# A fused attention, experts and feed-forward kernel: other orders in step 1 and of block sums, first weights loaded last, queries in one piece per head

## The reference

```
# attention: 2 sequences, 8 heads, 768 positions, 64 features
k_sum = k.reshape(B, H, 24, 32, D).max(axis=3)      # one summary key per block of 32
v_sum = v.reshape(B, H, 24, 32, D).mean(axis=3)
scores_l = scale * q @ k.T, where |i - j| < 16, else -1e9
scores_s = scale * q @ k_sum.T + log(32)
a = softmax(concat(scores_l, scores_s)); x = a @ concat(v, v_sum)
# four experts, 1536 tokens, 512 features, 1024 hidden
p = probs / (probs.sum(-1) + 1e-9)
x = sum_e p[:, e] * (relu(x @ w1[e]) @ w2[e])
# feed-forward, 2048 hidden
h = x @ w_in; out = (h * sigmoid(1.702 h)) @ w_out
```

## Time and profile before

| | us |
|---|---|
| three executions | 844.20, 845.85, 846.78 (median 845.85) |
| the profiled execution | 845.02 |
| its span | 843.2 |
| TensorE busy in it | 818.9 (97%) |
| VectorE / POOL / ACT busy | 542.0 / 555.5 / 399.1 |

### The profile page before, as it was taken

How to read it: one execution, slowest core, us unless ns; L and a number is a source line. 1 busy time by engine, 2 the same in 40 slices (tenths; PEclk the granted TensorE clock), 3 DMA queues, 4 the chain that set the end, 5 groups by cost and what they waited for, 6 DMA issues and landing times.

```text
span 843.2 us, 13851 instructions
## 1 busy us (share of the span) xinstructions
PE 818.9 (97%) x5014; PEld 805.1 (95%) x5014; DVE 542.0 (64%) x1194; ACT 399.1 (47%) x859; POOL 555.5 (66%) x414
## 2 busy tenths in 40 slices
PE   5896999999999999999999999999999999999998
PEld 4786999999999999999999999999999999999998
DVE  6896666656665566566566666666676665665665
ACT  3863544544444454434334344444455555454541
POOL 3685566656566699756656578877578887466450
PEclk9978999999999999999999999999999999999999
DMA  9981216142112112212213112112112112322102
GB/s 265 277 218 57 92 54 216 51 149 73 51 63 108 51 51 93 77 51 98 72 51 108 62 51 101 51 50 101 51 51 101 50 55 96 126 68 84 51 1 76
DMA packets 26420, 74.72 MB, mean 89 GB/s; under 512 B 14704, under 2 KB 15856, under 8 KB 20208
## 3 DMA queue, kind: packets, MB, share of 16 engines
q1 hardware_dynamic: 26352, 73.84, 26.9%
HBM read 70.66 MB, written 3.17 MB: 88 GB/s over the span
## 4 chain that ended last, share of the span: by engine, by line
PE 89%; POOL 3%; SPq 3%; issue 1%; DMA 1%; DVE 1%; ACT 1%; DVEq 0%; ACTq 0%; POOLq 0%
PE bank L1146 29%; PE bank L1148 29%; PE bank L1147 29%; DMA v_cols<-v_t 1%; PE bank L1101 1%; SPq L404 1%; PE bank L1138 1%; PE bank L1112 1%; SPq L411 1%; POOL wd_lo L543 0%; POOL wd_lo L559 0%; POOL xb_other_lo L567 0%; POOL w_sum L520 0%; SPq L422 0%; SPq L417 0%
## 5 line engine op out<-in xcount | busy, mean ns | idle before, releaser
L948 DVE TENSOR_TENSOR xa<-bank,xa 128x384 f32<-128x384 f32 x352 | 195.8, 557 | 220.0 <-PE bank L1148 215.6
L1146 PE MATMUL bank<-h_hi,wd_hi 128*128 128x384 f32 x768 | 257.8, 336 | 0.1
L1148 PE MATMUL bank<-h_lo,wd_hi 128*128 128x384 f32 x768 | 257.4, 335 | 0.0
L1147 PE MATMUL bank<-h_hi,wd_lo 128*128 128x384 f32 x768 | 257.3, 335 | 0.0
L543 POOL TENSOR_TENSOR wd_lo<-stage,wd_hi 128x1024 fp32r<-128x1024 f32 x47 | 112.5, 2393 | 169.1 <-ACT wd_hi L714 169.1
L755 ACT ACTIVATE h_hi<-bank 128x384 fp32r<-128x384 f32 x192 | 94.3, 491 | 226.0 <-DVE bank L981 178.7
L1146 PEld LDWEIGHTS bank<-h_hi,wd_hi 128*128 128x128 f32 x768 | 144.7, 188 | 1.2 <-issue 1.2
L1147 PEld LDWEIGHTS bank<-h_hi,wd_lo 128*128 128x128 f32 x768 | 144.7, 188 | 0.0
L1148 PEld LDWEIGHTS bank<-h_lo,wd_hi 128*128 128x128 f32 x768 | 144.7, 188 | 0.0
L531 POOL TENSOR_TENSOR wu_lo<-stage,wu_hi 128x1024 fp32r<-128x1024 f32 x47 | 112.6, 2396 | 0.0
L1146 PE MATMUL bank<-xb_other_hi,wu_hi 128*128 128x384 f32 x336 | 112.3, 334 | 0.3 <-ACT snap L739 0.3
(11 more groups left out here) (79 smaller groups left out, 1283.2 us busy)
## 6 DMA issues: line engine op xcount, KB each, us to landing
stage<-weights SPq DMA_DIRECT2D x48, 1024.0 KB, 4.9
k_win<-k_w SPq DMA_DIRECT2D x8, 720.0 KB, 8.9
v_win<-v_w SPq DMA_DIRECT2D x8, 576.0 KB, 9.1
q_bd<-q_t SPq DMA_DIRECT2D x16, 192.0 KB, 8.8
p_bc<-p_rows SPq DMA_DIRECT2D x8, 384.0 KB, 4.8
v_cols<-v_t SPq DMA_DIRECT2D x6, 384.0 KB, 6.0
out<-xa SPq DMA_DIRECT2D x4, 384.0 KB, 7.5
out<-xa SPq DMA_DIRECT2D x8, 192.0 KB, 1.9
```

The source lines that it names most:

```text
L948: nc.vector.tensor_tensor(at, y_bank(g, t), at, ALU.add).then_inc(y_taken, 1)
L1146: nc.tensor.matmul(dst, w_h, a_h, start=first, stop=False, skip_group_check=True)
L1147: nc.tensor.matmul(dst, w_l, a_h, start=False, stop=False, skip_group_check=True)
L1148: return nc.tensor.matmul(dst, w_h, a_l, start=False, stop=last, skip_group_check=True)
```

## The change

**Queries in one piece.** `q_bd` is laid out as [partition, column, tile] in place of [partition, tile, column], and the host stores `q_t` likewise. A half is then 3072 bytes in one piece for each of 64 partitions, where it was twelve pieces of 256 bytes. The 128 columns of a tile, which the score matmul loads, now lie 12 words, 48 bytes, apart. The zeroing is of the same size.

**Weights.** `load_weights(0)` goes behind unit 3's value columns and windows.

**Value sums.** For units 1 to 3 `value_sums`, `turn_value_sums` and `value_means` come one slot later (`values_due`), the spread in the same slot as before.

**First blocks and weights.** `high_raw(0)` goes from slot 10 to 12, `high_down(0, .)` from 13 to 14; POOL's halves of `wu_lo` from slots 11 and 12 to 13 and 14, those of `wd_lo` from slots 14 and 15 to behind `low_sums(1)`.

**Step 1.** ACT takes `keep(1, 1)` before the exponentials of group 12 and `high_raw(2)` behind the hidden tile; VectorE does `low_moved(4)` before `add_c11` and `value_sums(4)` behind the first `take_y`.

```
-            q_bd[i] = sb(stack, f"q_bd{i}", [P, TILES, P])
+            q_bd[i] = sb(stack, f"q_bd{i}", [P, P, TILES])
...
+        def values_due(slot, lag):
+            return [u for u in range(KT) if slot - lag == GROUPS * u + L_SUM + (u > 0)]
...
-                    sp.dma_start(q_bd[at_set(u)][rows, :, DH * half:DH * (half + 1)],
-                                 q_t[u, rows, :].rearrange("p (t n) -> p t n", n=QT)).then_inc(q_in[at_set(u)], 16)
+                    sp.dma_start(q_bd[at_set(u)][rows, QT * half:QT * (half + 1), :],
+                                 q_t[u, rows, :].rearrange("p (n t) -> p n t", t=TILES)
+                                 ).then_inc(q_in[at_set(u)], 16)
...
-            load_weights(0)
             load_value_columns(3)
             load_value_windows(3)
+            load_weights(0)
...
-                for u in unit_starting(slot, L_MEAN + 1):
-                    if u == 0:
-                        spread_value_means(u, kwin_done, 2)
-                for u in unit_starting(slot, L_MEAN + 2):
+                for u in values_due(slot, 2):
                     if u:
                         spread_value_means(u, norm_done, slot - L_NORM + 1)
-                if slot in (11, 12):
-                    low_first(slot - 11)
-                if slot in (14, 15):
-                    low_first(slot - 12)
+                    else:
+                        spread_value_means(u, kwin_done, 2)
+                if slot in (13, 14):
+                    low_first(slot - 13)
...
+                if g == 0:
+                    low_first(2)
+                    low_first(3)
                 if g + 1 < STEPS:
                     low_down(g + 1)
...
-                for u in unit_starting(slot, L_MEAN):
+                for u in values_due(slot, 1):
                     value_means(u)
-                if slot == 10:
+                if slot == 12:
                     high_raw(0)
-                if slot == 12:
                     high_moved(0, 0)
                 if slot == 13:
                     high_moved(0, B12)
+                if slot == 14:
                     high_down(0, 0)
                     high_down(0, 1)
...
                     high_down(1, 1)
+                    keep(1, 1)
                     exponent(B_GROUPS)
+                    high_hidden(1, "C11")
+                    high_moved(0, 5)
+                    high_raw(2)
...
             sum_first(4)
+            low_moved(4)
...
                     take_y(0, 0)
-                    low_moved(4)
+                    value_sums(KT)
+                    take_y(0, 1)
                     low_hidden(1, "C11")
-                    take_y(0, 1)
                     invert_sums(B_GROUPS)
                     take_y(0, 2)
                     low_moved(5)
                     take_y(0, 3)
-                    value_sums(KT)
...
-                    last = nc.tensor.matmul(s_bank(k)[:, t * KEYS:(t + 1) * KEYS], q_bd[at_set(u)][:, t0 + t, :],
+                    last = nc.tensor.matmul(s_bank(k)[:, t * KEYS:(t + 1) * KEYS], q_bd[at_set(u)][:, :, t0 + t],
```

More of the change, by code:

```diff
@@ L486, in _ @@
             for s in range(SETS):
-                nc.gpsimd.memset(q_bd[s][0:DH, :, DH:P], 0.0).then_inc(q_zeroed, 1)
+                nc.gpsimd.memset(q_bd[s][0:DH, QT:P, :], 0.0).then_inc(q_zeroed, 1)
             def spread_key_maxima(u):
@@ L795, in _ @@
                     high_down(1, 1)
+                    keep(1, 1)
                     exponent(B_GROUPS)
[L797 to L803, removed]
-                        exponent(k)
[L805 to L809, removed]
+                    high_hidden(1, "C11")
+                    high_moved(0, 5)
+                    high_raw(2)
+                else:
+                    if more:
+                        high_raw(g + 1)
+                    if ffn:
+                        sigmoid(g, "C11")
+                    high_hidden(g, "C11")
+                    for k in step_group(g):
+                        exponent(k)
+                    for k in step_group(g - 1):
+                        take_x(k)
+                    keep(g, 1)
                 if more:
@@ L995, in _ @@
             for s in range(SETS):
-                nc.vector.memset(q_bd[s][DH:P, :, 0:DH], 0.0).then_inc(q_zeroed_low, 1)
+                nc.vector.memset(q_bd[s][DH:P, 0:QT, :], 0.0).then_inc(q_zeroed_low, 1)
             for slot in range(SLOTS):
@@ L1008, in _ @@
                     key_maxima(u)
-                for u in unit_starting(slot, L_SUM):
+                for u in values_due(slot, 0):
                     value_sums(u)
@@ L1319 @@
         "consts": constants(),
-        "q_t": features_first(q),
+        "q_t": np.ascontiguousarray(features_first(q).reshape(UNITS, P, TILES, QT).swapaxes(2, 3)).reshape(UNITS, P, SEQ),
         "k_w": np.pad(windows(k_rows), ((0, 0), (0, 0), (0, 0), (0, NBLK))),
```

## The result

| | before | after |
|---|---|---|
| four executions each, us | 844.20 to 846.78, median 845.61 | 857.15 to 858.49, median 857.75 |
| ratio after / before | | 1.0145, interval 1.0126 to 1.0163 |
| the profiled execution, its span | 845.02, 843.2 | 857.26, 855.5 |
| TensorE busy | 818.9 | 838.8 |
| DMA packets | 26420 | 15156 |

A forecast was written before the change was run, and what follows sets the result against it. TensorE bounds everything behind 100 us, so gains lie before, the largest in its 5.26 us hole at P7. Step 1 -6.7, attention -1.4, stride 0: -8.1 us, giving 837.8 us from the median 845.85, range 835.2 to 844.0.

The forecast's parts named there:

- R3: Score matmuls: a strided load takes four times the packed one, 220 ns; +5.9 us, 851.8 us, slower; chance 9%.
- (a): Step 1: with keep(1,1) ahead of the exponentials and block 4's low part earlier, TensorE's hole at P7 goes; -5.4 us.
- (b): Step 1: 18 matmuls after the hole run at 0.17 instead of 0.33 us if the clock stays up; -2.7 us.
- (c): Step 1: value_sums(4) behind the first take_y removes TensorE's wait for it; -1.5 us.
- (d): Step 1: new TensorE waits for VectorE's take_y and POOL's normalization; +2.9 us together, between 1.4 and 4.5.
- (e): Step 1: POOL's wd_lo halves moved behind low_sums(1) cost 0 with 2 us of cover, up to 2 if landing is slow.
- (h): Attention: load_weights(0) behind unit 3's values lets value columns land earlier and the sum no longer delay mask 9; -1.8 us.
- (g): Attention: value sums of units 1 to 3 one slot later; +0.7 us, between 0 and +1.9.
- (f): Attention: queries in one piece let the first value columns land earlier; -0.7 us, between 0 and -2.8.
- (i): End of attention: low_first(1) of wu_lo behind POOL's last normalization ends at 47.7 us, covered by 1 us.
- (j): First tiles, begun 1.8 us earlier, may run that long at half clock rate; +0.4 us, between 0 and +0.9.
- R1: The clock falls all the same, a late landing of (e) counted here; gain only -4.9 us, 841.0 us; chance 17%.

The follow-up runs named there:

- run 6: The kernel before with only the change's step 1 orders of ACT and VectorE; 838.30 us, ratio 0.9925.
- run 7: The kernel before with all of the change but the queries' layout and the step 1 orders; 845.46 us, ratio 1.0003.
- Run 9: The kernel before with the step 1 orders and load_weights(0) behind unit 3's values, high_raw(0) staying in slot 10; 838.42 us.
- run 8: The changed kernel with query columns 8 bytes apart and the value sums of units 1 to 3 back in their old slots; 838.14 us.
- run 11: Run 6's kernel plus POOL's normalization of group 12 ahead of low_raw(2); 835.63 us, ratio 0.9878.
- run 1: The changed kernel with the old, packed layout of the queries, all new orders kept; 838.25 us, ratio 0.9924.
- run 12: Run 1's kernel plus POOL's normalization of group 12 ahead of low_raw(2); 836.61 us, ratio 0.9887.
- run 5: The changed orders with query columns 12, 24, 4 and 48 bytes apart in the four query buffers; 848.29 us in a single execution.
- run 3: The changed kernel with tiles in pairs, query columns 8 bytes apart, pieces of 512 bytes; 838.57 us.

## Why the prediction was wrong

**The step that failed** is the cost of the strided load, in one sentence: "I take 0, because the nearest rows leave half of the pace free." The half was free: packed, 32 lines at 1.8 ns are 58 ns (an estimate), near the 55 that the prediction drew from the 64-column loads. But the stride multiplies that time by four and more, not by up to two. The bound above, 220 ns, was a fair account of words coming one at a time (231 ns at 16 bytes, 219 at 24) and too low for 48 bytes (263). So the truth lay outside both ends, with 152 ns over the pace instead of 109: 14.6 us behind 50 us instead of 10.5, and 5.4 in attention instead of 3.5 (the last by one trace of each). The prediction's own sign of being wrong came: the loads pace at 263 ns, over its 130. Rival R3 named the mechanism and got 9%; it crossed to the slower side from 174 ns on, and of the steps tried only 4 and 8 bytes stay below that. With no row for or against, the four-fold bound, the only value that followed from a mechanism, deserved more than 9%.

**Step 1** was right: -6.7 foreseen, 6.7 us in run 6. (a) holds: no wait for `snap` at P7. (b) holds: clock 1.00 from 60 to 80 us (0.75 from 55 to 60, as the first tile begins). (c) holds: no wait for `v_sum`. (d) had the right engines and the wrong shares: VectorE 0.7 us in two waits (2.2 foreseen in four), POOL's `prob` 1.4 (0.7 foreseen), together 2.1 against 2.9. The sum came out though its shares did not: from the scores of group 12 to those of group 13 run 6 takes 20.9 us where before took 27.4, 6.5 less, and (a), (b) and (c) are worth 9.6, so 3.1 us were lost anew; what the waits do not show lies in short gaps beside them. In the changed kernel the waits are 0.2 and 1.4, since VectorE has 1.2 us more while TensorE loads group 12. (e) cost nothing: TensorE waits from 55 us to the end for VectorE's `xa`, POOL's `prob` and one `snap`, for no weights, and POOL's sums of step 2 do not wait for `stage`.

**Attention**, -1.4 foreseen, gave nothing: run 7 has 845.46 against 844.98. (h), -1.8, is not in run 7's time, though VectorE's wait for value columns at 34 us is gone there: its first tile starts at 49.66 us, between the 50.52 and 48.36 of the old orders. Before, that wait does stand in the chain of work that ended last, so the prediction had a path right; what it left out is that another must be about as long. Which one was not followed up. Run 9 adds little here, since its edit makes ACT wait 2.47 us for the weights. (g), +0.7, is not measurable (run 8). (f), -0.7: the packets came out (15156), and VectorE begins the first sum at 8.76 us in place of 9.47 in the changed kernel. That is no gain there, since TensorE leads, and within scatter: with the old layout it began at 9.24 in run 9 and 9.08 in run 11. Here one trace is worth little: the first tile starts at 50.52 us in the profiled execution of before and at 48.36 in that of run 6, whose instructions up to there are the same. (i) looked at the second half of `wu_lo` only. The first now stands ahead of the last normalization and holds it up: 3.8 us between the last two in place of 2.5 (the rows under the result, and the same in runs 1 and 7), with TensorE waiting 2.35 us behind. The move also frees earlier slots, and no run has the halves of `wu_lo` alone in their old slots, so what it costs in sum is open; it may be a part of what attention did not gain. (j) is within the scatter of the first tile's start and stays open.

The sum without the stride, -8.1, measured -6.3 (run 1), and R1 did not come.

From the first tile to the scores of group 13 the changed kernel and run 1 take 32.07 us alike, although the strided block of group 12 adds 1.2 us. VectorE's waits give back 0.5 (0.7 to 0.2), and the short gaps beside them about as much again: all that TensorE's starts between the two groups' scores lie over their 0.174 us pace is 3.2 us in run 1 and 2.2 in the changed kernel, the waits counted. The last 0.2 us is within the scatter.

## What to carry over

Lay out a stationary operand so that at least two of its 4-byte columns share 16 bytes, and cost any wider step by the lines that it touches, load by load, wherever TensorE leads. Before an operand's layout is changed for the sake of its transfer, ask which engine reads it and how often: here 192 loads paid for sixteen transfers. And a snapshot or a normalization for which TensorE waits belongs ahead of work that nobody wants yet; run 6 got 6.7 us from the snapshot and what went with it, runs 12 and 11 another 1.7 and 2.3 from the normalization.

## What was not expected of the hardware

A load of 128 columns costs about 1.8 ns for each 16-byte line it touches, 2.1 at 48 bytes. This price does not double where TensorE's clock halves. In run 5 the same 24-byte loads came at a granted clock of 0.50 (1.2 GHz) and of 1.00 (2.4 GHz). The windows:

```profile
15.00:17.00 2.00, 1.24 (x6) 1.27 (x6) 2.00 (x9) 1.85 (x11) 1.94 (x3) 0.50 0.97 254
21.40:23.40 2.00, 2.00 (x13) 2.00 (x11) 2.00 (x4) 0.90 (x5) 0.64 (x2) 1.00 1.06 295
```

and the loads in the first of them, to be held beside the row at 21.39 us above (1.85):

```profile
15.73 1.86 PEld L1113 LDWEIGHTS bank<-k_win,q_bd 128*128 128x128 f32 x8 [2.18 <-DMA q_bd<-q_t]
```

In run 3 eight loads at 8 bytes take 1.78 us where the clock is 0.50 and 1.02 where it is 1.00: there the matmul sets the pace. The granted clock does not tell all of it, though: before, eight packed loads also take 1.78 us at 15.81 us,

```profile
15.81 1.78 PEld L1101 LDWEIGHTS bank<-k_win,q_bd 128*128 128x128 f32 x8 [1.90 <-DMA q_bd<-q_t]
```

where the granted clock in the trace is 1.00 already, and 0.97 us from 21.56 us on. Why was not looked into. The 48-byte loads of the changed kernel take 2.21 us in both stretches.

Nor do larger pieces help in every form. Until 36 us the kernel with 512-byte pieces (run 3) moved 254 GB/s:

```profile
DMA packets 5137, 9.15 MB, mean 254 GB/s; under 512 B 479, under 2 KB 3679, under 8 KB 5087
```

where those with 256-byte pieces moved 280 before and 277 to 299 in runs 6 and 7, and that with 3072-byte pieces 296 after; 8 bytes and 48 bytes apart differ in the writes as well, so this does not say what the length of a piece alone is worth.
